# Where the turned attention blocks land: 2048-byte rows or 448-byte runs

## The reference

```python
scores = cap * tanh(q @ k.T / 8 / cap)            # per head, 448 x 448, cap = 30
attn   = exp(scores - max(scores)); attn /= sum(attn) + 1e-9
x      = (attn @ v), heads side by side           # 1792 x 768
x      = (sigmoid(x @ w_gate) * (x @ w_val)) @ w_out      # d_ff 1536
h      = x @ w_in;  y = (h * cos(h)) @ w_out2             # d_ff 2048
```

## Time and profile before

| what | value |
|---|---|
| median of three runs | 1219.19 us |
| the profiled execution | 1217.53 us |
| its span (first to last instruction) | 1215.6 us |
| PE busy | 1201.2 us, 99% |
| VectorE, ScalarE, POOL busy | 626.0, 508.8, 516.4 us |
| DMA packets, bytes | 119314, 304.67 MB |

### The profile page before, as it was taken

One profiled execution on the slowest core, in us unless ns is written; L12 is line 12 of the kernel. 1 busy time (PEld: TensorE's weight loads), 2 busy tenths in 40 slices (PEclk: granted clock), 3 DMA queues, 4 the chain that ended last, 5 costly groups with the idle time before them and its releaser, 6 DMA issues.

```text
span 1215.6 us, 16763 instructions
## 1 busy us (share of the span) xinstructions
PE 1201.2 (99%) x5932; PEld 1090.0 (90%) x5932; DVE 626.0 (51%) x1226; ACT 508.8 (42%) x957; POOL 516.4 (42%) x458
## 2 busy tenths in 40 slices
PE   8999999999999999999999999999999999999998
PEld 6779999999899999888999999999999999999998
DVE  8951158866763456766651266777662111105610
ACT  8941155655641454545641145545661011105510
POOL 7969968789653346662103406664301100000000
PEclk8999999999999999999999999999999999999999
DMA  4579986799777699999678769899768566666663
GB/s 159 162 244 322 326 304 228 254 328 325 266 265 255 218 270 273 266 278 278 239 238 282 255 212 297 273 280 272 268 233 288 199 215 223 211 216 223 241 230 109
DMA packets 119314, 304.67 MB, mean 251 GB/s; under 512 B 17472, under 2 KB 26432, under 8 KB 119232
## 3 DMA queue, kind: packets, MB, share of 16 engines
q1 hardware_dynamic: 111024, 291.80, 72.1%
q10 hardware_dynamic: 8208, 11.81, 3.3%
HBM read 219.39 MB, written 58.98 MB: 229 GB/s over the span
## 4 chain that ended last, share of the span: by engine, by line
PE 91%; DMA 2%; SPq 2%; ACT 2%; DVE 2%; issue 1%; ACTq 0%; POOL 0%; POOLq 0%
PE acc L825 25%; PE acc L827 25%; PE acc L826 25%; PE s_ps L723 3%; PE s_ps L724 2%; PE acc L778 2%; DMA pt_lo_whole<-h_lo_whole 2%; PE t_ps L795 1%; SPq L466 1%; PE t_ps L760 1%; PE t_ps L797 1%; PE t_ps L744 1%; PE acc L815 1%; DMA w_hi<-w_pair 1%; PE acc L817 1%
## 5 line engine op out<-in xcount | busy, mean ns | idle before, releaser
L825 PE MATMUL acc<-h_hi,w_hi 128*128 128x448 f32 x672 | 247.4, 368 | 0.2 <-DMA w_hi<-w_pair 0.2
L826 PE MATMUL acc<-h_lo,w_hi 128*128 128x448 f32 x672 | 245.6, 366 | 0.0
L827 PE MATMUL acc<-h_hi,w_lo 128*128 128x448 f32 x672 | 245.5, 365 | 0.0
L825 PE MATMUL acc<-x_hi,w_hi 128*128 128x448 f32 x576 | 210.9, 366 | 0.0
L826 PE MATMUL acc<-x_lo,w_hi 128*128 128x448 f32 x576 | 210.6, 366 | 0.0
L827 PE MATMUL acc<-x_hi,w_lo 128*128 128x448 f32 x576 | 210.6, 366 | 0.0
L544 POOL TENSOR_TENSOR pt_lo<-pt_lo_whole,pt_hi 128x1344 fp32r<-128x1344 f32 x24 | 74.6, 3110 | 229.0 <-ACT pt_hi L1048 229.0
L825 PE MATMUL acc<-z_hi,w_hi 128*128 128x448 f32 x384 | 140.6, 366 | 1.2 <-DMA w_hi<-w_pair 1.1
L827 PE MATMUL acc<-z_hi,w_lo 128*128 128x448 f32 x384 | 140.4, 366 | 0.0
L826 PE MATMUL acc<-z_lo,w_hi 128*128 128x448 f32 x384 | 140.4, 366 | 0.0
L825 PEld LDWEIGHTS acc<-h_hi,w_hi 128*128 128x128 f32 x672 | 126.3, 188 | 10.5 <-DMA w_hi<-w_pair 0.6
(11 more groups left out here) (137 smaller groups left out, 1984.3 us busy)
## 6 DMA issues: line engine op xcount, KB each, us to landing
w_lo<-w_pair SPq DMA_DIRECT2D x156, 384.0 KB, 4.0
w_hi<-w_pair SPq DMA_DIRECT2D x156, 384.0 KB, 3.3
w_lo_whole<-w SPq DMA_DIRECT2D x52, 384.0 KB, 3.7
w_pair<-w_lo SPq DMA_DIRECT2D x52, 384.0 KB, 4.2
w_pair<-w_hi SPq DMA_DIRECT2D x52, 384.0 KB, 4.8
w_lo<-w_pair SPq DMA_DIRECT2D x36, 512.0 KB, 4.5
w_hi<-w_pair SPq DMA_DIRECT2D x36, 512.0 KB, 3.6
qk_in_whole<-qk SPq DMA_DIRECT2D x35, 512.0 KB, 6.2
```

The source lines that it names most:

```text
L825: e.matmul(out[:, 0:S], w_hi[u % HI][:, wb, :], a_hi[:, kb, :], start=first, stop=False)
L826: e.matmul(out[:, 0:S], w_hi[u % HI][:, wb, :], a_lo[:, kb, :], start=False, stop=False)
L827: return e.matmul(out[:, 0:S], w_lo[u % LO][:, wb, :], a_hi[:, kb, :], start=False, stop=last)
```

## The change

The DMAs land the blocks directly in the plain form of `pt_lo`: chunk by chunk, head by head, with the 448 queries of a head in a row. For each key block a run of 112 elements (448 bytes, one head's queries of one quarter in one chunk) is moved. A DMA has 4 runs in each of its 32 partitions for r = 2 and 3, and 3 for r = 0 and 1. The unused fourth block and the 16 unused elements of each block are no longer moved. The part of the buffer that no DMA writes any more is cleared once at the start, so `PADS` is one larger. The views `head_blocks` and `by_quarter` go.

```diff
-PADS = 1 + 2 + 2
+PADS = 1 + 2 + 1 + 2
...
-    lows, lows_whole = sb_both("pt_lo", [P, 2 * 4 * SLOTS * SLOTS * QB])
-    pt_lo = lows[:, 0:CH * 2 * S].rearrange("p (c s) -> p c s", c=CH)
-    last_prob = lows_whole[:, CH * 2 * S:CH * 2 * S + S].rearrange("p (t s) -> p t s", t=1)
+    pt_lo, pt_whole = sb_both("pt_lo", [P, CH + 1, 2 * S])
+    last_prob = pt_whole[:, CH:CH + 1, 0:S]
...
+    def chunks_in(r):
+        return CH + (r in LAST_KEYS)
+    def blocks_to(pr, d, i, r):
+        rows, own = slice(QB * i, QB * (i + 1)), slice(QB // 2 * d, QB // 2 * d + QUARTER)
+        blocks = turned_blocks(pr, d).rearrange("p (k x) -> p k x", x=SLOTS * QB)
+        return blocks[rows, FIRST_KEYS[r]:FIRST_KEYS[r] + chunks_in(r), own]
+    def landing(d, i, r):
+        first = S * d + QUARTER * i
+        return pt_whole[QB * r:QB * (r + 1), 0:chunks_in(r), first:first + QUARTER]
...
                     for r in range(4):
-                        at, n = SLOTS * QB * FIRST_KEYS[r], SLOTS * QB * (CH + 1)
-                        to = pb_whole[QB * r:QB * (r + 1), d, i, :, :].rearrange("p c x -> p (c x)")
-                        e.dma_start(to, turned_blocks(pr, d)[QB * i:QB * (i + 1), at:at + n]).then_inc(s_moved[d], 16)
+                        e.dma_start(landing(d, i, r), blocks_to(pr, d, i, r)).then_inc(s_moved[d], 16)
...
-                whole, low, at = head_blocks(d, pb_whole), head_blocks(d, pb_lo), of_head(d)
-                rest(low[:, :, 0:CH, :], whole[:, :, 0:CH, :], by_quarter(pt_hi[:, 0:CH, at])).then_inc(s_pblow, 1)
+                at = of_head(d)
+                rest(pt_lo[:, 0:CH, at], pt_whole[:, 0:CH, at], pt_hi[:, 0:CH, at]).then_inc(s_pblow, 1)
...
-                        e.matmul(out, vv, head_blocks(d, pb_lo)[:, :, c, :], start=False, stop=False)
+                        e.matmul(out, vv, pt_lo[:, c, of_head(d)], start=False, stop=False)
...
-                e.activation(by_quarter(pt_hi[:, :, of_head(d)]), head_blocks(d, pb_whole), ACT.Copy).then_inc(s_pbhi, 1)
+                e.activation(pt_hi[:, :, of_head(d)], pt_whole[:, :, of_head(d)], ACT.Copy).then_inc(s_pbhi, 1)
...
+            e.memset(pt_whole[0:D, CH, S:2 * S], 0.0).then_inc(s_pad, 1)
```

More of the change, by code:

```diff
@@ L147, in build @@
     x_pair = scratch[:, 4, :]
-    pb_lo, pb_whole = (t.rearrange("p (d i c x) -> p d i c x", d=2, i=4, c=CH + 1) for t in (lows, lows_whole))
     turned_h = [h_hi_whole[:, OF_H:OF_H + SLOTS, :], h_lo_whole[:, OF_H:OF_H + SLOTS, :]]
@@ L610, in moved_low @@
                 e.wait_ge(s_pbhi, 2 * (pr - MOVED) + d + 1)
-                whole, low, at = head_blocks(d, pb_whole), head_blocks(d, pb_lo), of_head(d)
-                rest(low[:, :, 0:CH, :], whole[:, :, 0:CH, :], by_quarter(pt_hi[:, 0:CH, at])).then_inc(s_pblow, 1)
+                at = of_head(d)
+                rest(pt_lo[:, 0:CH, at], pt_whole[:, 0:CH, at], pt_hi[:, 0:CH, at]).then_inc(s_pblow, 1)
                 e.wait_ge(s_pblow, 2 * (pr - MOVED) + d + 1)
-                last = slice(CH, CH + 1)
-                rest(by_quarter(pt_hi[0:D, last, at]), whole[D:P, :, last, :],
-                     by_quarter(pt_hi[D:P, last, at])).then_inc(s_pb, 1)
+                rest(pt_hi[0:D, CH, at], pt_whole[D:P, CH, at], pt_hi[D:P, CH, at]).then_inc(s_pb, 1)
                 e.wait_ge(s_pb, 2 * (pr - MOVED) + d + 1)
@@ L1055, in move_last_blocks @@
                 for r in range(4):
-                    at, n = SLOTS * QB * FIRST_KEYS[r], SLOTS * QB * (CH + 1)
-                    to = pb_whole[QB * r:QB * (r + 1), d, 3, :, :].rearrange("p c x -> p (c x)")
-                    e.dma_start(to, turned_blocks(pr, d)[QB * 3:P, at:at + n]).then_inc(s_moved[d], 16)
+                    e.dma_start(landing(d, 3, r), blocks_to(pr, d, 3, r)).then_inc(s_moved[d], 16)
             def all_moved(pr):
```

## The result

The changed kernel takes 1212.47 us (median of four runs, 1211.97 to 1212.74) against 1219.43 us for the kernel before beside it (four runs, 1216.98 to 1221.9). The ratio is 0.9942, 95% interval 0.9922 to 0.9963: faster by 0.6%. Two later measurements of twelve runs each, on two chips, gave 0.9957 (0.9942 to 0.9973) and 0.9961 (0.9948 to 0.9975). So the gain is 4.5 to 7 us. The forecast was a loss of 12.5 us. Rival A had the sign, but its price stopped at 3.9 us.

What follows compares the result with a forecast made beforehand. PE, busy 1201.2 of 1215.6 us, was the bound, with DMA near capacity in two stretches. Added DMA time of 8.6 and 3.9 us reaching PE, others 0, gave +12.5: 1232 us, own range 1224 to 1242, overall 1216 to 1262.

Steps and rivals of the forecast that it cites:

- Rival A: Moves in the loaded stretches: short runs cost nothing extra, engines pay by the byte; 1215 to 1219 us, chance 24%.
- The two loaded stretches: 440 to 580 and 740 to 860 us, stages 1 and 2 with moved heads: DMA busy 0.94 and 0.96, at capacity's edge.
- the path from landing to ScalarE to the score bank to PE: First stretch, 440 to 580 us: slow landings hold up ScalarE 24.9 us and PE's weight load 3.6 us for the tanh.
- POOL (3099 against 3111 ns): POOL's strided subtraction: plain views aren't dearer or cheaper, so 0, with +-0.3 us a head.
- SP's issue: Issue of a move on SP, 592 ns: value 0, as the number of rows doesn't set it.
- PE's 365 and 368 ns: PE's products of low parts, 365 ns through the view, 367 plainly: 0 over 72 products, at most 0.15 us.
- the hidden clear: Clear at the start, 0.42 us of VectorE, covered by 2.19 us idle before its first subtraction; +0.4 us if uncovered.
- 3.5 runs are 133 ns: +30.5 ns a row: DMA time of a move's row: 3.5 runs of 38.1 ns replace a 2048-byte row of 103 ns.
- the line: Packet price through the mean packets of q1 and q10: 0.0405 ns per byte and 20 ns per packet.
- the chain has no slack and I count all 8.6: First stretch, 440 to 580 us: PE already stands for landings, so all 8.6 us of added DMA time reach PE.
- Its condition: Rival A decides from the point where a run costs under 103 / 3.5 = 29 ns.
- Its cap of 3.9 us: Rival A can win only PE's idle time in the two loaded stretches, 3.8 + 0.07 = 3.9 us.

Runs made afterwards that it cites:

- The runs of 512 bytes: Kernel before, same 2048 bytes a row landed as four 512-byte runs, buffer ordered chunk first, views still strided: 1220.07 us, ratio 1.0023.
- the padded one: Changed kernel plus an unused 2048 bytes a partition behind its landing buffer, so later tensors keep their old addresses: 1212.13 us, ratio 0.9958.
- the strided kernel with PE's plain operand: 448-byte runs in the old buffer, but 72 PV products read the high parts plainly instead of the low parts through the strided view: 1214.45 us, 0.9974.
- the changed kernel with jumps: Changed kernel, but the same 72 products read a head's low parts in runs of 112 in another order: 1213.55 us, ratio 0.9960.

## Why the prediction was wrong

**Where it was right.** The two loaded stretches are the place; in the first, the path from landing to ScalarE to the score bank to PE is the one on which the profile's time moved (24.9 to 15.5 us of ScalarE's waits, 3.6 us of PE's weight load for the tanh gone). The counts of packets and bytes hold. POOL (3099 against 3111 ns), SP's issue (602 against 592 ns; the minimum rose from 507 to 585), PE's 365 and 368 ns and the hidden clear (0.43 us, where 0.42 was said) came as priced.

**The step that failed: "3.5 runs are 133 ns: +30.5 ns a row".** Measured: 3.5 x 32.7 = 114 ns against 125 for the long row, -11 ns. Both ends of the line were off: the line gave 38.1 ns to the run (measured 32.7, 19 ns a row) and 103 ns to the row (measured 125, 22 ns). A line through the mean packet of two queues is no price list: each queue's mean includes tiny packets (17345 records of 4 bytes, 10 ns each), and the long packets of the moves grew by half under load. From the packet records themselves the quiet prices are 16, 24, 27 and 84 ns for 256, 448, 512 and 2048 bytes: near 8 ns and 0.037 ns a byte, no step at 512 bytes. The sum follows: 12288 x 11 / 16 = 8.4 us of DMA time less, where 23.4 more were forecast. The Trainium skill, "DMA: Bandwidth & Descriptors", Specifications, would have a penalty under 512 bytes, and the same page's section "Why small descriptors are slow (HBM only)" exempts SBUF to SBUF. The quiet prices of 256, 448 and 512 bytes lie on one line with that of 2048, so no step shows at 512 bytes here, as the exemption has it; a fixed part of about 8 ns a packet does show.

**A second step failed: "the chain has no slack and I count all 8.6".** In no run did added DMA time reach PE at that rate. The runs of 512 bytes added 19.9 us of DMA time, nearly the 23.4 of the forecast, and brought both stretches to shares of 0.99 and 1.00. They lost 2.8 us (0.23%, interval 0.06 to 0.41%), not 12.5. So the size of the forecast was wrong too, and not only its sign.

**Rival A had the sign, and its terms failed too.** Its condition was a run under 103 / 3.5 = 29 ns; the run takes 32.7, and it was the dearer row, 125 ns, that put the point of balance at 36. Its cap of 3.9 us was read from PE's idle time. A matmul is shown for 366 ns while the next starts 203 ns after it, so each stall shows 0.16 us too short. Where starts of successive matmuls lie over 0.22 us apart, what they exceed 0.203 us by sums to 5.1 us of stalls in the first stretch before and 0.2 after; PEld's busy time gives 5.0 for the difference. The whole difference of the two profiles (4.9 us of span) is there. The runs of the kernel before also spread more (1212.4 to 1224.2 over 35 runs in one group, 1211.1 to 1214.6 over twelve of the changed one), so its profile shows one course among several.

**What is shown of the cause, and what is open.** Shown: in the old buffer, the time rises with the DMA time of a row. 106 and 108 ns give 0.9984 and 0.9990, 119 to 125 ns 0.9990 to 1.0001, 151 ns 1.0023, 200 ns 1.0103. The plain form has two points that agree with this: 114 to 116 ns give 0.996, 138 ns 0.9997. The two forms don't lie on one line. Shown also: in this kernel the runs alone (0.9999 and 1.0001 in one kernel, 0.9991 and 0.9990 in two of its kind) give nothing that can be told, and the plain form with four runs neither (0.9997); both together, with three or four runs, give 0.4% (0.9957, 0.9961, and 0.9958 and 0.9958 in the padded one and the one without the clear). Whether the plain form would gain as much at the load of before was not tried, so a gain of the form that simply adds to that of the load isn't ruled out. The addresses behind the buffer, the distance of the runs and the clear are ruled out.

**A part of it is PE's pace, not stalls.** Two things in a profile differ from one kernel to the next: gaps of over 0.22 us between the starts of matmuls, and the pace within the rest (last section). Taking from each span what the gaps and the pace have beyond 202.7 ns a matmul leaves 1176.1 to 1177.1 us in all twenty profiles. The five profiles of the changed kernel average 1210.1 us and the four with strided runs of 448 bytes 1214.9. Of the 4.9 us between them, gaps are 2.7 and pace is 2.2. The pace part is 2.3 to 2.6 us in the plain profiles without jumps and 3.1 to 5.8 in the old buffer, but for the one of the kernel before (2.7); with a clear added that kernel has 4.4. So the gain between before and changed in the first pair of profiles is nearly all stalls, while the difference of the two forms is to nearly a half pace, which DMA time isn't shown to set.

Not settled: which plain view carries it. PE's view restored half in one direction and took nothing in the other; ScalarE's and POOL's views were not tried alone, and their own durations don't differ. That the engines' reads disturb the landing writes is only a guess, for which the mean of 34 against 33 ns a packet (old buffer against plain) is thin support. So the cause of the form's share stays open. No version beat the changed kernel by more than the noise.

## What to carry to other kernels

Price a packet by records of its own size class, in the quiet and under load, and not by a queue's mean. Here, with the DMA engines busy over 0.9 of the time, bytes and packets both counted: in the same buffer, trimmed rows in one piece gained 0.2%, runs of 448 bytes with still fewer bytes nothing, and the same bytes in four or eight packets lost 0.2% and 1%. A load that is nearly at the limit isn't yet one that PE pays in full: +20 us of DMA time cost 2.8. Take the cap on what stalls can give back from the weight-load side or from starts of matmuls, not from PE's idle time, and change run and layout apart before crediting either.

## What the runs showed of the hardware that was not expected

PE has two paces with the granted clock at 1.00 and no wait. From one matmul to the next it is 202.7 ns on average (a mixture near 199, 203 and 207) or 206.6 steadily, and it keeps a pace for tens of us. Windows 100 to 160 us, the same work in both, first the strided kernel with PE's plain operand, then the changed kernel with jumps:

```profile
100.00:160.00 60.00, 60.00 (x298) 55.59 (x297) 11.27 (x18) 10.43 (x20) 55.58 (x49) 1.00 0.93 324
```

```profile
100.00:160.00 60.00, 60.00 (x293) 54.52 (x292) 11.28 (x18) 9.63 (x17) 55.69 (x48) 1.00 0.94 320
```

298 against 293 matmuls in 60 us, before any moved block exists. The slow pace cost the second kernel 1.1 us there (293 x 3.9 ns). Of the thirteen profiles with the old buffer three had it in this stretch, of the seven with the plain one this one. After the last moved head of batch 2 (near 860 us) eleven of the thirteen had it and none of the seven; the kernel before, in its one profile, and the strided one with PE's plain operand were the two without. Up to the moved heads all these kernels run the same instructions but for the clear. What sets the pace was not found.
